# Six projections per head instead of eight, and a new order of side work: hashed attention, a bilinear block and four gated experts on one core

## The reference

```python
q_bits = (einsum('bhsd,dk->bhsk', q, proj) > 0)        # proj: 64 x 6, the same for k
mask = q_bucket[:, :, :, None] == k_bucket[:, :, None, :]
scores = where(mask, q @ k.T / sqrt(D), -1e9)
attn_out = softmax(scores) @ v                         # heads side by side: x, 1536 x 512
a, b = x @ w1, x @ w2                                  # 512 x 1024 each
x = (a * b @ w3) @ w_out
out = sum_e p[:, e] * (relu(x @ w1[e]) @ w2[e])        # 4 experts, 512 -> 1024 -> 512
```

## Time and profile before

| | us |
|---|---|
| median of 3 runs | 1004.42 |
| lowest and highest run | 1004.26, 1005.74 |
| the profiled execution | 1004.14 |
| its span | 1002.4 |

### The profile page before, as it was taken

How to read it: one execution, slowest core, us unless ns; L and a number is a source line. 1 busy time by engine, 2 the same in 40 slices (tenths; PEclk the granted TensorE clock), 3 DMA queues, 4 the chain that set the end, 5 groups by cost and what they waited for, 6 DMA issues and landing times.

```text
span 1002.4 us, 15929 instructions
## 1 busy us (share of the span) xinstructions
PE 992.5 (99%) x5526; PEld 922.1 (92%) x5526; DVE 638.8 (64%) x964; ACT 460.9 (46%) x853; POOL 410.5 (41%) x416
## 2 busy tenths in 40 slices
PE   9999999999999999999999999999999999999998
PEld 6889999999989999999998998989989899898997
DVE  6359999999997996498755353453634536345342
ACT  4248888888875553455552240422404224042230
POOL 4022424385467992594254160431604316043130
PEclk9999999999999999999999999999999999999999
DMA  6323343333333220011010110101101011010102
GB/s 242 95 72 103 96 118 94 94 102 107 90 86 83 74 66 22 22 43 43 8 57 22 43 43 9 56 22 43 43 14 50 21 42 42 19 44 21 42 17 109
DMA packets 58925, 60.58 MB, mean 60 GB/s; under 512 B 7808, under 2 KB 46848, under 8 KB 58880
## 3 DMA queue, kind: packets, MB, share of 16 engines
q1 hardware_dynamic: 58880, 60.00, 20.0%
HBM read 44.20 MB, written 3.19 MB: 47 GB/s over the span
## 4 chain that ended last, share of the span: by engine, by line
PE 89%; DVE 6%; issue 2%; ACT 2%; DMA 1%; POOL 0%; SPq 0%; DVEq 0%; ACTq 0%; POOLq 0%
PE ps L290 22%; PE ps L291 22%; PE ps L292 22%; PE ps L1394 6%; PE ps L1381 3%; PE ps L1409 3%; PE ps L1411 3%; PE ps L1383 3%; PE ps L1359 2%; PE ps L1354 2%; DVE w_lo L1023 2%; DVE hid_lo L1149 1%; DMA w_raw<-in_moe_w 1%; DVE pT_lo L1008 1%; PE ps L1313 1%
## 5 line engine op out<-in xcount | busy, mean ns | idle before, releaser
L617 POOL TENSOR_TENSOR v_sum<-kept,kept 128x384 f32<-128x384 f32 x48 | 52.0, 1083 | 291.6 <-ACT kept L803 291.6
L1281 DVE SCALAR_TENSOR_TENSOR acc<-ps,gate,acc 128x512 f32<-128x512 f32 x96 | 72.0, 750 | 134.4 <-PE ps L292 134.4
L803 ACT COPY kept<-ps 128x384 f32<-128x384 f32 x144 | 64.0, 481 | 195.8 <-PE ps L292 195.0
L292 PE MATMUL ps<-v_hi,hid_lo 128*128 128x512 f32 x384 | 149.6, 390 | 0.0
L291 PE MATMUL ps<-v_lo,hid_hi 128*128 128x512 f32 x384 | 149.5, 389 | 0.0
L290 PE MATMUL ps<-v_hi,hid_hi 128*128 128x512 f32 x384 | 149.4, 389 | 0.0
L990 DVE TENSOR_SCALAR_CACHE_REDUCE expo<-ps 128x768 f32<-128x768 f32 x96 | 91.7, 955 | 15.9 <-PE ps L1383 15.6
L705 ACT ACTIVATE expo<-expo,neg_max 128x768 f32<-128x768 f32 x96 | 90.7, 945 | 7.2 <-DVE expo L990 5.7
L1268 DVE SCALAR_TENSOR_TENSOR hid_lo<-c,hid_hi 128x384 fp32r<-128x384 f32 x96 | 64.5, 685 | 46.2 <-ACT hid_hi L924 19.1
L713 ACT CAST pT_hi<-ps 128x768 fp32r<-128x768 f32 x96 | 76.9, 803 | 32.7 <-PE ps L1394 32.4
L1008 DVE TENSOR_TENSOR pT_lo<-ps,pT_hi 128x768 fp32r<-128x768 f32 x96 | 90.4, 946 | 1.1 <-ACT pT_hi L713 1.1
(11 more groups left out here) (160 smaller groups left out, 2514.4 us busy)
## 6 DMA issues: line engine op xcount, KB each, us to landing
w_raw<-in_moe_w SPq DMA_DIRECT2D x64, 128.0 KB, 2.4
e_raw<-in_moe_w SPq DMA_DIRECT2D x64, 128.0 KB, 2.3
v_raw<-in_moe_w SPq DMA_DIRECT2D x32, 256.0 KB, 3.2
w_raw<-in_moe_w SPq DMA_DIRECT2D x8, 512.0 KB, 4.2
raw_q<-in_q SPq DMA_DIRECT2D x16, 192.0 KB, 2.9
raw_k<-in_k SPq DMA_DIRECT2D x16, 192.0 KB, 2.9
raw_v<-in_v SPq DMA_DIRECT2D x16, 192.0 KB, 2.7
q_main<-q_cross SPq DMA_DIRECT2D x16, 192.0 KB, 2.7
```

What stands on the lines that cost most here:

```text
L292: return nc.tensor.matmul(out_ps, lhs_lo, rhs_hi, start=False, stop=stop, skip_group_check=onto)
L617: nc.gpsimd.tensor_tensor(v_sum[:, :], kept[s][1][:, :], kept[s][2][:, :], ALU.add).then_inc(v_done, 1)
L803: nc.scalar.copy(kept[s][n][:, :], ps[4 * s + n][:, 0:HALF]).then_inc(kept_done, 1)
L1281: nc.vector.scalar_tensor_tensor(acc[:, t, :], ps[4 * ((h + t // 4) % 2) + t % 4], gate_f[:, bass.ds(t * E + e, 1)], acc[:, t, :], ALU.mul ...
```

## The change

- `prep` with j = 4 has two matmuls (one per half) in place of four with the low part of proj: POOL copies the high part of q (rows 0 to 63 of q_cross) and of k (rows 64 to 127 of k_cross) into q_main (`stack_highs`, two copies of 64x768), and one weight tile holds the low part of proj for both. The four matmuls with the high part are in `project_parts`. In a body these come where prep 4 was; prep 4 comes after `score(1, 2)`. The low part of proj is no longer multiplied with the low parts of q and k.
- `move_high` has one DMA less, since q_main's upper rows come from POOL; `stacks_moved` counts 48 per head.
- DVE's `encode(2, 4)` comes after `scale(1, 2)`.
- POOL's order in a body: splits of q and k, of v, `stack_highs`, then `x_scale`, then `first_parts`. The steps of `first_parts` are spread from the fifth pair to the last one, the first of them (-1) holding two of the four sums.
- `gates` on ACT: `next_gate_rest(a)` and the kept copies of step a+1 come before the copy to a11.
- Experts: ACT copies the high part of w2 pieces after the first and the second kept copy of steps 2 and 3; POOL's `split_v2` comes ahead of its sum of kept tiles; DVE's `sum_c12` comes ahead of the third `low`, with waits for PE to match.

```diff
-    V2_IN_STEP = ((), (0, 1), (2, 3), ())
+    V2_IN_STEP = ((), (), (0, 1), (2, 3))
...
-        proj_w = [place(f"proj_w{n}", [P, P], F32R, prep_at) for n in range(8)]
+        proj_w = [place(f"proj_w{n}", [P, P], F32R, prep_at) for n in range(6)]
...
-                move(s, (q_main[s][0:DH, :], q_cross[s][0:DH, :]), (k_main[s][0:DH, :], k_cross[s][DH:P, :]))
+                move(s, (k_main[s][0:DH, :], k_cross[s][DH:P, :]))
...
+            def stack_highs(m, s, values):
+
+
+                pool.wait_ge(v_split, values)
+                for part, (rows, src) in enumerate(((slice(0, DH), q_cross), (slice(DH, P), k_cross))):
+                    pool.wait_ge(prep_copied, 4 * m + 2 * part + 2)
+                    held()
+                    nc.gpsimd.tensor_copy(q_main[s][rows, :], src[s][rows, :].bitcast(F32)).then_inc(highs_stacked, 1)
+                    pool.wait_ge(highs_stacked, 2 * m + part + 1)
...
-                if step == 0:
+                if step == -1:
                     pool.wait_ge(x_scaled, 2 * DK)
                     nc.gpsimd.tensor_tensor(s_raw[:, 0, :, :], x[:, low, t1], x[:, high, t1], ALU.add).then_inc(xf_done, 1)
                     nc.gpsimd.tensor_tensor(s_raw[:, 2, :, :], x[:, low, t0], x[:, low, t1], ALU.subtract)\
                         .then_inc(xf_done, 1)
+                elif step == 0:
...
-                    for t in range(TILES):
-                        if t == 0 and not last:
-                            split_q(m + 2, i + 1, s, False)
-                        if t == 1 and not last:
-                            split_k(m + 2, s)
-                        if t in (2, 4) and s == 0 and not first:
-                            x_scale(i - 1, t // 2 - 1)
-                        if t == 3 and s == 0:
-                            split_v(m + 1, i, 1, first)
-                        if t == 3 and s == 1 and not last:
-                            split_v(m + 1, i + 1, 0, False)
-                    for step in parts[s:s + 1]:
-                        for n in step:
+                    if last and s == 0:
+                        for n in parts:
+                            first_parts(n)
+                    if not last:
+                        split_q(m + 2, i + 1, s, False)
+                        split_k(m + 2, s)
+                    if s == 0:
+                        split_v(m + 1, i, 1, first)
+                    elif not last:
+                        split_v(m + 1, i + 1, 0, False)
+                    if not last:
+                        stack_highs(m + 2, s, m + 2)
+                    if s == 0 and not first:
+                        x_scale(i - 1, 0)
+                        x_scale(i - 1, 1)
+                    if parts and not last:
...
-            attention(DK, False, False, ((0,), (1, 2)))
-            attention(DK + 1, False, False, ((3,), (4,)))
-            attention(DK + 2, False, False, ((5,), (6, 7)))
-            attention(PAIRS - 1, False, True)
+            attention(DK, False, False, ((), (-1,)))
+            attention(DK + 1, False, False, ((0,), (1, 2)))
+            attention(DK + 2, False, False, ((3,), (4, 5)))
+            attention(PAIRS - 1, False, True, (6, 7))
...
+                        for p in V2_IN_STEP[j]:
+                            split_v2(ROUNDS * e + h, p)
                         sum_kept(step, (h + j) % 2)
                         pool.wait_ge(hid_lo_done, 4 * unit)
                         last_quarter(step, c22)
                         if first and h == 0:
                             clear(j)
-                        for p in V2_IN_STEP[j]:
-                            split_v2(ROUNDS * e + h, p)
...
+            def keep(step, s, pieces=(), r=0):
                 for n in range(3):
                     act.wait_ge(prod, N_PROD * step + n + 1)
                     nc.scalar.copy(kept[s][n][:, :], ps[4 * s + n][:, 0:HALF]).then_inc(kept_done, 1)
+                    for p in pieces[n:n + 1]:
+                        act.wait_ge(v2_loaded[p], 16 * r + 16)
+                        nc.scalar.copy(v2_hi[p][:, :], v2_raw[p][:, :]).then_inc(v2_hi_done, 1)
...
+                    next_gate_rest(a)
+                    keep(a + 1, 1)
                     if unit:
                         act.wait_ge(hid_lo_done, 4 * unit - 1)
                     act.wait_ge(prod, N_PROD * a + 6)
                     nc.scalar.copy(a11[:, :], ps[BANK_A][:, 0:HALF]).then_inc(a11_done, 1)
-                    next_gate_rest(a)
-                    keep(a + 1, 1)
...
+                    scale(1, 2)
                     encode(2, 4)
-                    scale(1, 2)
...
-                    nc.vector.tensor_copy(proj_w[2 * n][:, cols[n]], proj_f[:, :]).then_inc(proj_hi_ready, 1)
+                    nc.vector.tensor_copy(proj_w[n + n // 2][:, cols[n]], proj_f[:, :]).then_inc(proj_hi_ready, 1)
                 dve.wait_ge(proj_hi_ready, 4)
                 for n in range(4):
-                    nc.vector.tensor_tensor(proj_w[2 * n + 1][:, cols[n]], proj_f[:, :],
-                                            proj_w[2 * n][:, cols[n]].bitcast(F32), ALU.subtract)\
+                    rows = slice(0, DH) if n % 2 == 0 else slice(DH, P)
+                    nc.vector.tensor_tensor(proj_w[3 * (n // 2) + 2][rows, cols[n]], proj_f[rows, :],
+                                            proj_w[n + n // 2][rows, cols[n]].bitcast(F32), ALU.subtract)\
...
+                        sum_c12(step, s, c12)
                         low(2, ps[4 * s + BANK_A][:, 0:HALF], B * f + b, t0)
-                        sum_c12(step, s, c12)
...
-                elif 1 <= j <= 4:
+                elif 1 <= j < 4:
...
-                    for n, w in enumerate(proj_w):
-                        half = slice((n // 4) * HALF, (n // 4 + 1) * HALF)
-                        last = nc.tensor.matmul(ps_prep[:, 0:HALF], w[:, :],
-                                                (q_cross if n % 4 < 2 else k_cross)[s][:, half],
-                                                start=n == 0, stop=n == 7)
+
+                    pe.wait_ge(highs_stacked, 2 * m + 2)
+                    for h in range(2):
+                        last = nc.tensor.matmul(ps_prep[:, 0:HALF], proj_w[3 * h + 2][:, :],
+                                                q_main[s][:, h * HALF:(h + 1) * HALF], start=False, stop=h == 1)
...
+            def project_parts(m, s):
+
+                pe.wait_ge(prep_copied, 4 * m + 4)
+                for h in range(2):
+                    for n, src in enumerate((q_cross, k_cross)):
+                        nc.tensor.matmul(ps_prep[:, 0:HALF], proj_w[3 * h + n][:, :],
+                                         src[s][:, h * HALF:(h + 1) * HALF], start=h + n == 0, stop=False)
...
-                    pe.wait_ge(stacks_moved[s], 64 * (i + 1))
+                    pe.wait_ge(stacks_moved[s], 48 * (i + 1))
...
-                    prepare(2, 4)
+                    project(2)
                     if last and s:
                         gate_products(0, (1,))
                     transpose(5)
                     score(1, 2)
+                    prepare(2, 4)
...
+                            pe.wait_ge(hid_lo_done, 4 * up_unit(e, h, j - 2) + 3)
...
+                            pe.wait_ge(hid_lo_done, 4 * up_unit(e, h, 2 if t == 0 else 3) + 3)
```

More of the change, by code:

```diff
@@ L422, in _ @@
             move_onehots(HEADS - 1, 1)
-            sp.wait_ge(stacks_moved[1], 64 * PAIRS)
+            sp.wait_ge(stacks_moved[1], 48 * PAIRS)
             sp.wait_ge(prep_mm, GROUPS * HEADS)
@@ L507, in _ @@
             nc.gpsimd.memset(ident[:, :], 0.0).then_inc(zeros_set, 1)
-            for n in range(8):
+            for n in range(6):
                 nc.gpsimd.memset(proj_w[n][:, :].bitcast(F32), 0.0).then_inc(zeros_set, 1)
@@ L516, in _ @@
             split_v(0, 0, 0, True)
+            for s in range(2):
+                stack_highs(s, s, 1)
             def first_parts(step):
@@ L550, in attention @@
                     m = 2 * i + s
-                    for t in range(TILES):
-                        if t == 0 and not last:
-                            split_q(m + 2, i + 1, s, False)
-                        if t == 1 and not last:
-                            split_k(m + 2, s)
-                        if t in (2, 4) and s == 0 and not first:
-                            x_scale(i - 1, t // 2 - 1)
-                        if t == 3 and s == 0:
-                            split_v(m + 1, i, 1, first)
-                        if t == 3 and s == 1 and not last:
-                            split_v(m + 1, i + 1, 0, False)
-                    for step in parts[s:s + 1]:
-                        for n in step:
+                    if last and s == 0:
[14 more added lines that the diff above has]
+                    if parts and not last:
+                        for n in parts[s]:
                             first_parts(n)
@@ L797, in _ @@
             o_lower(2 * HEADS - 1, ps_prep)
-            def keep(step, s):
```

(15 more changed lines are left out.)

4 lines of the change are left out of this document (3 added, 1 removed).

## The result

The changed kernel takes 993.24 us (median; 992.96 to 995.03) against 1004.26 us for the kernel before beside it: a ratio of 0.9893, with a 95% interval of 0.9879 to 0.9908. 993.9 had been forecast, within 991.0 to 998.2. The profiled execution of after took 992.96 us, with a span of 991.2 (before: 1004.14 and 1002.4), so the span to explain is 11.2 us.

The account below looks back on a forecast made before the run. TensorE, busy 99% of the span, was taken as the bound. Savings of 4.2 + 0.45 + 2.25 - 0.15 + 1.4 + 2.35 = 10.5 us gave 993.6 against the profiled execution, 993.9 in the median; range 991.0 to 998.2.

Parts of the forecast that it names:

- Bound: Whole kernel: TensorE busy 99% of the span, the next engine 64%; DVE and ACT close behind in the attention loop.
- Two matmuls per head: Attention loop: 0.35 us less TensorE work per head, 0.05 lost waiting at `score(1, 2)`; 14 x 0.30 = 4.2 us saved.
- First two heads: Prologue: head 0 saves 0.35 us, head 1 loses 0.25 of its 0.35; together 0.45 us (0.35 to 0.7).
- Copies of POOL: Loop, before prep 4: new 64x768 copies take 0.83 us each; room 1.4 us, so TensorE does not wait.
- Slow bodies: Three loop bodies where POOL's subtraction holds up `guarded`: each loses its 0.75 us excess, 2.25 us saved.
- Last pair: Last pair of heads: `x_scale` comes where `guarded` stands, but DVE leads there; 0.15 us lost (0 to 1.8).
- Gates: Gates: kept copies no longer wait behind a11; 0.70 us in batch 0 and 0.70 in batch 1, together 1.4 us saved.
- experts: Experts, step 3: second kept copy comes earlier; 0.25 us in each of 7 rounds and 0.6 in the eighth, 2.35 saved.
- DVE in TensorE's place: Rival, attention loop: DVE's releases and score chain set the pace, the 14 heads give nothing; 998.1 us, chance 0.07.
- the blocked guard: Rival, loop: q's copy takes 1.84 us and holds `guarded`, about 0.65 us in each of 14 bodies; 1003.0 us, chance 0.05.
- POOL at prep 4: Rival, loop: TensorE waits for POOL's k copy from 2.2 us on; at 4 us 1019 us; chance 0.04.
- the side orders do nothing: Rival, gates and experts: both gain 0 because POOL's or DVE's pace is behind the kept copies; 997.7 us, chance 0.05.

Follow-up runs that it names:

- e5b: Changed kernel with POOL's stacking copy of q made a longer subtraction of the tile from itself: 998.56 us, 0.9951 of the kernel before.
- e1: Changed kernel with two more matmuls per head, by a tile of zeros, added to the four projections: 998.18 us, 0.9937 of the kernel before.
- e6: Changed kernel with POOL's copy of k made four times: 1023.68 us, 1.0190 of the kernel before.
- e2: Kernel before without `guarded`, the DVE addition of EPS to the row sums: 1002.63 us, 0.9979 of the kernel before.
- e10: Kernel before, eight projections kept, with POOL's new order of splits, `x_scale` and x parts but without the stacking copies: 1003.51 us, 0.9993 of the kernel before.
- e8: Changed kernel with x parts one place earlier and, in the last pair, `x_scale` of the first half ahead of v's split: 993.33 us, 0.9892 of before.
- e3: Kernel before with ACT's new order in the gates alone: 1003.06 us, 0.9984 of the kernel before.
- e4: Kernel before with the experts' new orders alone (w2 pieces, POOL's splits, DVE sums): 1001.91 us, 0.9975 of the kernel before.
- e11: Changed kernel run once more, unaltered, side by side with a variant on the same chip: 993.26 us (993.00 to 994.42), span 992.6.
- e7: Changed kernel with prep 4 directly behind the four projections and DVE's sign bits ahead of `scale(1, 2)`: 995.51 us, 0.9908 of the kernel before.

## Why the prediction was right, step by step

- **Bound.** TensorE before and after. The gain is what left its list (5.6 us) and its waiting (5.6 us), and the forecast had both.
- **Two matmuls per head**: forecast 4.2 us for 14 bodies, measured 4.9 (15.42 to 15.07). The estimated wait of 0.05 at `score(1, 2)` isn't there, since the way from release to matmul, put at 0.12 from the kept copies, is 0.06 at this place (e5b, and 0.06 in before's slow bodies): with that the prediction's own sum comes to 171.09, ahead of the 171.13 at which TensorE is ready. This is the largest error in us, 0.7, and 0.05 us of slack decided it. e1 gives the term back.
- **First two heads**: 0.45; head 1 does lose the 0.25 that was said: its gap before prep 4 is 0.316 us where a back-to-back one is 0.175, TensorE was released by POOL, and the second of the two matmuls starts 0.11 late.
- **Copies of POOL**: 0.82 and 0.83, taken as 0.83; room 1.4, measured 1.37, and e6 used it up. That the copies cost nothing because 1.4 us cover them is shown.
- **Slow bodies**: all three gone, and e2 shows the guard as their cause. Why they go was argued in one piece from the order on POOL; e10 splits it: one body goes by the spread, two by the copies that now stand between v's split and the parts. What the argument had not seen are the guards of 0.67 to 0.78 us in before's other second heads: that they too went, which the 4.9 us of the first term need, was luck.
- **Last pair**: the term furthest off for its size, 0.15 us against 0.53. I had seen `x_scale` come where the guard stands, and still took DVE's lead of before for granted; by e5b the lead is 0.1 us once four matmuls less stand ahead of `score(1, 2)`. It cost little in the end: by e8 POOL's weight chain would have taken it.
- **Gates** 1.4 against 1.51 (alone in e3: 1.36), **experts** 2.35 against 2.49 (alone in e4: 2.50). One short wait was said to stay in batch 0, and one does in the profiled execution. In e11's there are two, and the term is nothing: it holds in most executions, not in all. What the prediction said against counting the first wait, that POOL sets when the weights come, is what happens there.
- **Sum**: 10.5 forecast, 11.2 in the spans: 0.7 more from the loop, 0.1 each from gates and experts, 0.4 less from the last pair; the rest is the start.
- **Rivals**: DVE in TensorE's place was 0.1 us away, by e5b; the blocked guard came in none of the loop bodies, and in one of the last pair; POOL at prep 4 is excluded by the 1.4 us; that the side orders do nothing, by e3 and e4, except for the gates in e11's execution.

## What to carry to other kernels

When work goes from the bounding engine's list, or moves behind the place where it meets the next engine, that engine's lead there shrinks by all of it. Here two matmuls went and two moved, so from `scale(1, 1)`'s end to `score(1, 2)` the 0.80 us of before became 0.11, with 0.45 in e1 and 0.60 in e7, where six stand ahead. Take every delay that was hidden before and set it against the new lead, not the old (here 0.74 us hidden with eight matmuls ahead, 0.1 with four), and read the small instruction in every kind of body, not in one. Where a small instruction is long in some bodies and short in others, look at what the other engine runs when it ends, and separate the two by what stands between them. Before a local wait is mended, follow the chain to the next place where the engine meets the same supplier: e8 mended 0.54 us and found it again 10 us later.

## What the runs showed of the hardware that I had not expected

- POOL's cast costs the same for half the partitions: 0.82 to 0.83 us at 64x768, 0.83 at 128x768. Its subtraction doesn't: 1.46 us at 64x768 against 1.84 at 128x768 (the first reads one tile twice, so the operands differ too; which of the two does it was not tried).
- DVE's 128x6 addition waits for the end of POOL's two-input instruction (1.81, 0.91, 0.74 and 0.70 us in place of 0.17), but its 128x6 reciprocal, SBUF to SBUF as well, doesn't: 0.19 us in e2 while POOL casts, and 0.17 in after, while POOL subtracts:

```profile
288.19 0.72 POOL L587 TENSOR_TENSOR w_raw<-w_raw 128x256 f32<-128x256 f32 x1
```
```profile
288.76 0.17 DVE L1018 RECIPROCAL row_rec<-guarded 128x6 f32<-128x6 f32 x1
```

- The addition waits for the end of POOL's copy too: in after it takes 0.21 to 0.25 us in the four second heads in which the copy ends 0.18 to 0.21 us behind its start, and 0.15 to 0.17 in the other bodies of the loop.
- Two copies of POOL on one tile, of which the second waits for the first's semaphore, start 1.0 us apart: 0.17 us go to that wait.
